# Padding rows of the expert table issued by GpSimd behind its last row scatters, instead of by SyncE between row loads and weight loads

## What is computed

```
def _moe2_ref(x, expert_emb, tau, w1, w2):
...
    logits = xn @ en.T / tau
    expert_idx = np.argmax(logits, axis=1)
...
    for e in range(E):
        mask = expert_idx == e
...
        h = np.maximum(x[mask] @ w1[e], 0.0)
        out[mask] = gate_w[mask, None] * (h @ w2[e])
```

## Time and profile before

| | |
|---|---|
| time, median of 3 runs | 955.76 us (955.58 to 956.93) |
| the profiled execution | 955.82 us, of it 953.8 us span |
| PE busy | 938.2 us, 98% |
| DVE busy | 656.7 us, 69% |
| ACT busy | 305.1 us, 32% |
| POOL busy | 252.4 us, 26% |
| mean granted TensorE clock | 0.996 of full |
| DMA queue q1 (SP) | 120.51 MB |
| DMA queue q0 (POOL) | 12.61 MB |

### The profile page before, as it was taken

How to read it: one execution, slowest core, us unless ns; L and a number is a source line. 1 busy time by engine, 2 the same in 40 slices (tenths; PEclk the granted TensorE clock), 3 DMA queues, 4 the chain that set the end, 5 groups by cost and what they waited for, 6 DMA issues and landing times.

```text
span 953.8 us, 16202 instructions
## 1 busy us (share of the span) xinstructions
PE 938.2 (98%) x5680; PEld 797.0 (84%) x5680; DVE 656.7 (69%) x1157; ACT 305.1 (32%) x420; POOL 252.4 (26%) x192
## 2 busy tenths in 40 slices
PE   8999999999999999999999999999899999999996
PEld 7888888888888888888888888889799999888885
DVE  5656589747983698459965897777665557798641
ACT  4232121112111211112111222235455557678541
POOL 4453214341433143413432132421000001100101
PEclk9999999999999999999999999999999999999999
DMA  8432296024001500140002302178966667799611
GB/s 309 157 112 78 106 383 232 1 89 144 0 0 49 182 0 0 44 165 1 1 23 78 123 0 89 50 275 283 359 227 224 230 227 272 293 366 361 232 42 54
DMA packets 32754, 139.76 MB, mean 147 GB/s; under 512 B 5264, under 2 KB 5648, under 8 KB 23970
## 3 DMA queue, kind: packets, MB, share of 16 engines
q1 hardware_dynamic: 25186, 120.51, 34.9%
q0 software_dynamic: 4336, 12.61, 3.4%
q10 hardware_dynamic: 3168, 5.79, 1.9%
HBM read 126.27 MB, written 28.41 MB: 162 GB/s over the span
## 4 chain that ended last, share of the span: by engine, by line
PE 91%; DMA 4%; DVE 1%; SPq 1%; issue 1%; ACT 1%; ACTq 0%; POOLq 0%; DVEq 0%
PE bank L776 28%; PE bank L794 27%; PE bank L923 13%; PE bank L891 8%; PE bank L869 5%; DMA attention<-in_w_exp 3%; PE bank L662 2%; PE bank L706 2%; PE bank L678 2%; PE bank L695 1%; PE bank L761 1%; PE bank L902 1%; DVE weights_split L1294 1%; DMA expert_rows<-rows,slot_i 1%; SPq L428 1%
## 5 line engine op out<-in xcount | busy, mean ns | idle before, releaser
L776 PE MATMUL bank<-activations_split,weights_split 128*128 128x512 f32 x1152 | 277.6, 391 | 0.0
L794 PE MATMUL bank<-weights_split,activations_split 128*128 128x512 f32 x1152 | 276.2, 389 | 0.0
L794 PEld LDWEIGHTS bank<-weights_split,activations_split 128*128 128x128 f32 x1152 | 216.1, 188 | 45.0 <-POOL activations_split L1834 0.3
L776 PEld LDWEIGHTS bank<-activations_split,weights_split 128*128 128x128 f32 x1152 | 215.2, 188 | 45.8 <-issue 1.4
L1834 POOL TENSOR_TENSOR activations_split<-scratch,activations_split 128x512 fp32r<-128x512 f32 x84 | 123.5, 1471 | 304.4 <-ACT activations_split L1577 299.7
L1577 ACT CAST activations_split<-scratch 128x512 fp32r<-128x512 f32 x96 | 59.8, 623 | 411.6 <-DVE scratch L1067 400.8
L923 PE MATMUL bank<-weights_split,activations_split 128*128 128x512 f32 (+1 forms) x648 | 158.6, 396 | 0.0
L923 PEld LDWEIGHTS bank<-weights_split,activations_split 128*128 128x128 f32 x648 | 118.5, 188 | 23.2
L1062 DVE TENSOR_SCALAR scratch<-bank,alpha 128x512 f32<-128x512 f32 x96 | 71.7, 747 | 93.2 <-PE bank L776 92.5
L1294 DVE TENSOR_TENSOR weights_split<-attention,weights_split 128x2048 fp32r<-128x2048 f32 (+1 forms) x45 | 102.5, 2289 | 27.0 <-ACT weights_split L1657 26.4
L1892 POOL DMA_INDIRECT out<-scratch,y_token x27 | 31.9, 1182 | 272.9 <-ACT scratch L1690 272.3
(11 more groups left out here) (253 smaller groups left out, 741.7 us busy)
## 6 DMA issues: line engine op xcount, KB each, us to landing
attention<-in_w_exp SPq DMA_DIRECT2D x48, 1024.0 KB, 4.8
en_all<-in_w_exp SPq DMA_DIRECT2D x16, 1024.0 KB, 6.9
attention<-in_kv SPq DMA_DIRECT2D x43, 256.0 KB, 4.2
expert_rows<-in_pad_rows SPq DMA_DIRECT2D x8, 1285.0 KB, 25.2
rows<-in_w_mlp SPq DMA_DIRECT2D x14, 512.0 KB, 4.0
attention<-in_qk SPq DMA_DIRECT2D x12, 512.0 KB, 5.4
rows<-expert_rows ACTq DMA_DIRECT2D x22, 257.0 KB, 3.1
scratch<-in_qk SPq DMA_DIRECT2D x10, 512.0 KB, 3.9
```

What stands on the lines that cost most here:

```text
L776: last = mm(H_ps[f % 2][:, :], win(a, kc, f), x[:, kc, :], start=(k == 0), stop=(k == 3 * KC - 1))
L794: last = mm(bank[j][:, :], x[f % 2][:, j * P:(j + 1) * P], wout(a, f), start=(f == 0 and a == 0 and part_ == "hi"), stop=(f == FB - 1 and ...
```

## The change

The call of `pads` moves from SP's stream to POOL's.

```
@@ sync engine
                 r = sp.value_load(tab[0:1, T_PROW + 2:T_PROW + 3], min_val=0, max_val=PAD - 2 * P)
                 sp.dma_start(xrow[n][:, :], table[bass.ds(r + n * P, P), :]).then_inc(s_xld[n], 16)
-            pads(sp)
             half(2, 1)
             sp.wait_ge(s_pad0, due(s_pad0, 16))
             sp.wait_ge(s_pads, due(s_pads, 16 * E))
@@ gpsimd
             mlp(NC - 1, router_c=NC - 2)
             scatter(NC - 1)
+            pads(pool)
```

## The result

The changed kernel is slower: 961.37 us (median of 5 runs, 959.83 to 963.10) against 955.76, a ratio of 1.0058 with a 95% interval of 1.0043 to 1.0073. The forecast was 951.7. The wait that the change aims at is gone, and a wait more than twice as long stands elsewhere.

A forecast was written before the change was run, and what follows sets the result against it. PE bounds the kernel, with one real wait, 2.9 us for DVE's low half, laid to the pads on SP ahead of weight loads. 955.82 - 4.4 (stall) + 0.3 (tile 4's rows) = 951.7 us; 8-in-10 range 951.0 to 955.3.

The forecast's parts named there:

- rival A: Whole kernel: PE's stall in pair 2 goes and little comes in its place, 951.2 to 952.4 us; chance 58%.
- PE's wait for tile 4's rows: Tile 4's row load meets the pads in the DMA engines; PE waits 0 to 1.0 us, taken as +0.3.
- The stall removed, -4.4 us: Pair 2, fourth group: PE's 2.86 us wait and its slow clock go once SP issues parts 2 and 3 without pads ahead.
- POOL's time is hidden, DVE does not hold a pad, POOL does not hold DVE: Pads on POOL beside DVE's splits: idle POOL hides their time; holds taken as 0, keeping 9 us (POOL) and 1 us (DVE).
- At a pitch of 1.55 POOL has issued four pads by 650.3: POOL's pads ahead of tile 4's row load: four at a pitch of 1.55 us, three at 1.97.
- The row load issued at 650.26: SP issues tile 4's rows at 650.26; landing 655.8 to 657.2, wanted by PE at 656.17.
- The order in which the engines serve: DMA engines with SP's and POOL's transfers: service in order of issue, so tile 4's rows wait only for three or four pads.
- rival C: Tile 4's rows wait for nearly all pads as engines alternate packet by packet; PE waits 3.2 to 5.2 us, 956.1 to 958.1; 12%.
- Rival D: Pads end after 669.5, too late for SP's wait; each us beyond costs one, 952.5 to 955.5 us; chance 7%.

The follow-up runs named there:

- e4: Changed kernel with pads of 16 rows instead of 256, same eight issues on POOL without most bytes; 951.93 us, ratio 0.9956 to the kernel before.
- e8: e3 with SP's loads of parts 0 and 1 of pair 3 ahead of its wait for the pads; 951.81 us, ratio 0.9957 to the kernel before.
- e10: e2 with SP's loads of parts 0 and 1 of pair 3 ahead of its wait for the pads; 952.20 us, ratio 0.9954 to the kernel before.
- e7: Changed kernel with four pads behind the row scatters, four after tiles 4 and 5's rows landed; 952.83 us, ratio 0.9963 to the kernel before.
- e3: Changed kernel with POOL's pads issued once the row scatters have landed, together with tiles 4 and 5's row loads; 952.21 us, ratio 0.9968 to the kernel before.
- e6: Changed kernel with pads of the same bytes in small packets, 4112 B instead of 32,896 B; 958.14 us, ratio 1.0025 to the kernel before.
- e1: Changed kernel with POOL's pads issued only once the rows of tiles 4 and 5 have landed; 952.99 us, ratio 0.9967 to the kernel before.
- e2: Kernel before, pads still on SP but behind parts 2 and 3 of pair 2 instead of ahead; 953.27 us, ratio 0.9969 to the kernel before.
- e9: Changed kernel measured once more, without an edit; 960.94 us, ratio 1.0043 to the kernel before.

## Why the prediction was wrong

The forecast was rival A, 951.7 us, with a chance of 58%. It failed in one term, PE's wait for tile 4's rows, put at +0.3 and measured at 7.1, with 2.6 more for the slow clock behind it.

**The stall removed, -4.4 us.** Right. Pair 3 follows pair 2 after 23.39 us in the changed kernel, and e4, e8 and e10 give the gain in the time, 0.43% to 0.46%.

**POOL's time is hidden, DVE does not hold a pad, POOL does not hold DVE.** Right. Pads of 0.49 us stand at 648.30 and 649.43, within DVE's split of 647.77 to 650.06; the split starts 5.49 us behind its pair, as before.

**"At a pitch of 1.55 POOL has issued four pads by 650.3."** This is the step that failed. The pitch was 0.55 us for the first four and 1.13 for the rest, eight pads by 651.05. The 1.55 was SP's pitch plus the longer register load, added up as if load and issue took turns; on POOL the register loads of the first pads were done while earlier scatters were still running, and the pitch was given as the low end of the range. The number of pads ahead of tile 4's rows was thereby eight, and with four (e7) the forecast wait of 0 to 1.0 us was 1.12. With eight in place of four the prediction's own sum gives a landing at 649.5 + 8 x 1.42 + 2 = 662.9, a wait of 6.7 us; measured were 663.7 and 7.1. So nearly all of the wait is in the count.

**The row load issued at 650.26.** Missing in the sum: the row scatters themselves got the pads behind them in their own queue, and the last landed 8.34 us after its issue instead of 6.63. With the pads' bytes taken away (e4) SP issued the rows at 649.97 again. How much of the wait these 1.7 us are, no run separates: in e7 the rows were issued 2.4 us later than forecast and landed 0.6 behind the end of the forecast range.

**The order in which the engines serve.** The prediction read the 4 us without a packet of POOL's as service in the order of issue and held it against rival C. The runs show such a silence for either queue when the other has its work already lined up: before, POOL's scatter of 661.13 had its first packet at 666.11; in the changed kernel, SP's rows of 652.34 had theirs at 656.36. Behind it both move (76 to 85 packets). e3's part 3, overtaken by six pads issued after it, and e6's last three pads, overtaken by tile 4's rows, rule out the order of issue. What sets the length of the silence stays open.

**Rival C**, tile 4's rows behind nearly all pads, is what happened. It had 12%. Its price, 956.1 to 958.1, was too low: the wait was 7.1 us where it had 3.2 to 5.2, and the slow clock and the slow transpose cost 2.6 us where it took 1.5 from the shorter stall before.

**Rival D**, pads too late for SP's wait, did not come into play in the changed kernel, where everything behind PE's wait was late anyway. It is what kept e1 and e2 short of the full gain: SP passed the wait at 673.4 and 674.7, and pair 3 was 0.8 and 2.2 us late. In e3 SP passed it at 672.6, and what pair 3 was late there, 0.6 us, came from part 3 of pair 2 instead. So the point where it begins to cost is, by an estimate from these three, near 672.5, not 669.5.

## What to carry to other kernels

Moving bulk transfers to an idle engine frees the queue they leave, but what they then share with everyone is the DMA engines; the earlier they are issued, the more small urgent loads find them lined up ahead. Before such a move, list the short loads with little slack that are issued in the next 10 us, and count the bytes ahead of each, for the fastest issue that is possible, not for the pitch seen on the other engine. Bulk that nobody needs soon goes behind the urgent loads, on whatever queue, and the wait for it behind the next loads that don't need it.

## What the runs showed of the hardware

- A load that arrives while another queue has megabytes lined up can get no packet for some 4 us (issued at 652.34, first packet at 656.36; with nothing lined up 0.9 us), with packets of 32,896 B and of 4112 B alike (e6, first packet at 656.37). With four pads instead of eight ahead it was 1.3 us (e7, issued at 652.67, first packet at 654.01). Then both queues move packets, in counts of the same order (76 to 85 here, 123 to 88 in e3), whatever was issued first.
- GpSimd issued plain DRAM to DRAM transfers of 514 KB in 0.49 to 0.58 us each: 0.55 apart for the first four of the changed kernel, whose register loads had run ahead, and 1.13 apart for the others there and in e3.
- The same 7 us wait was followed by a different stretch at 1.2 GHz in two runs of the same kernel: the 24 matmuls behind it took 7.83 us in the first and, here in e9's timeline of PE, 6.89 (in e6, behind 7.2 us, 7.11):

```profile
664.53 6.89 PE L922 MATMUL bank<-weights_split,activations_split 128*128 128x512 f32 x24
```
